# Output transposes moved from the matrix engine to 32 by 32 squares on VectorE, and half of the squarings moved to ScalarE

## What is computed

```python
out = np.einsum('hk,bskhg->bshg', softmax(weight), x_unf)      # 7 taps, causal
x1  = (sigmoid(x @ w_gate) * (x @ w_val)) @ w_out              # d_ff 1536
h   = x1 @ w_in2;  r = np.maximum(h, 0);  y = (r * r) @ w_out2 # d_ff 2048
```

## Time and profile before

| | |
|---|---|
| median of 3 executions | 2421.84 us |
| profiled execution, whole | 2421.73 us |
| profiled execution, span of the trace | 2419.5 us |
| TensorE busy | 2387.3 us, 99% |
| VectorE busy | 1824.4 us, 75% |
| ScalarE busy | 1162.6 us, 48% |
| GpSimd busy | 174.6 us, 7% |
| TensorE's granted clock, mean | 0.998 |

### The profile page before, as it was taken

How to read it: one execution, slowest core, us unless ns; L and a number is a source line. 1 busy time by engine, 2 the same in 40 slices (tenths; PEclk the granted TensorE clock), 3 DMA queues, 4 the chain that set the end, 5 groups by cost and what they waited for, 6 DMA issues and landing times.

```text
span 2419.5 us, 54234 instructions
## 1 busy us (share of the span) xinstructions
PE 2387.3 (99%) x20880; PEld 1942.8 (80%) x20880; DVE 1824.4 (75%) x3468; ACT 1162.6 (48%) x2208; POOL 174.6 (7%) x164
## 2 busy tenths in 40 slices
PE   6999999999999999999999999999999999999998
PEld 5788888888888888888888888888888888888886
DVE  6777777777777777877777777778777777777755
ACT  3544544454544444544545444445445444454544
POOL 3300000000000000000000000000000000000010
PEclk9999999999999999999999999999999999999999
DMA  5211111111111101111111111111111111111110
GB/s 131 60 47 28 39 48 30 46 28 41 46 42 36 45 22 46 48 30 46 28 41 46 31 45 36 33 46 48 30 46 28 39 48 30 46 28 41 40 38 19
DMA packets 99902, 99.41 MB, mean 41 GB/s; under 512 B 8736, under 2 KB 86048, under 8 KB 99872
## 3 DMA queue, kind: packets, MB, share of 16 engines
q1 hardware_dynamic: 99856, 98.99, 16.7%
q10 hardware_dynamic: 16, 0.00, 0.0%
HBM read 19.27 MB, written 12.58 MB: 13 GB/s over the span
## 4 chain that ended last, share of the span: by engine, by line
PE 98%; DVE 1%; ACT 0%; issue 0%; DMA 0%; POOL 0%; SPq 0%; ACTq 0%; DVEq 0%
PE hp L400 53%; PE acc L466 25%; PE acc L471 17%; PE hp L401 1%; DVE y L815 1%; PE acc L467 0%; PE hp L506 0%; PE acc L472 0%; DMA stage<-in_moe_w_val_dram 0%; PE hp L515 0%; POOL wo L358 0%; DVE hid_t L767 0%; DMA moved<-z_parts 0%; SPq L263 0%; ACT xT L637 0%
## 5 line engine op out<-in xcount | busy, mean ns | idle before, releaser
L400 PE MATMUL hp<-xs,w 64*128 64x512 f32 x5760 | 1413.2, 389 | 13.6 <-DVE hid_t L767 5.3
L401 PE MATMUL hp<-xs,w 64*128 64x512 f32 x5760 | 1413.2, 389 | 0.0
L400 PEld LDWEIGHTS hp<-xs,w 64*128 64x128 f32 x5760 | 1061.7, 185 | 256.1 <-DVE hid_t L767 7.3
L401 PEld LDWEIGHTS hp<-xs,w 64*128 64x128 f32 x5760 | 1061.7, 185 | 0.0
L781 DVE TENSOR_TENSOR lo<-hid_t,hi 128x512 fp32r<-128x512 f32 x896 | 615.4, 687 | 7.9
L771 DVE TENSOR_TENSOR hid_t<-act_t 128x512 f32<-128x512 f32 x512 | 384.7, 752 | 246.1 <-ACT act_t L628 246.1
L625 ACT ACTIVATE act_t<-hp 128x512 f32<-128x512 f32 x384 | 229.9, 599 | 689.4 <-PE hp L400 689.3
L467 PE MATMUL acc<-hi,wo 64*128 64x512 f32 x1792 | 560.7, 393 | 0.0
L466 PE MATMUL acc<-hi,wo 64*128 64x512 f32 x1792 | 560.7, 393 | 0.0
L767 DVE TENSOR_TENSOR hid_t<-hp,act_t 128x512 f32<-128x512 f32 x384 | 265.0, 690 | 261.7 <-ACT act_t L625 253.3
L628 ACT ACTIVATE act_t<-hp 128x512 f32<-128x512 f32 x512 | 302.8, 598 | 310.6 <-PE hp L401 310.6
(11 more groups left out here) (69 smaller groups left out, 1890.3 us busy)
## 6 DMA issues: line engine op xcount, KB each, us to landing
xs<-xs SPq DMA_DIRECT2D x160, 256.0 KB, 3.8
xs<-y_rest SPq DMA_DIRECT2D x128, 128.0 KB, 3.1
out_dram<-stage SPq DMA_DIRECT2D x32, 384.0 KB, 2.6
xin<-in_x_dram SPq DMA_DIRECT2D x30, 384.0 KB, 4.3
moved<-y_parts SPq DMA_DIRECT2D x32, 128.0 KB, 2.2
moved<-z_parts SPq DMA_DIRECT2D x64, 64.0 KB, 2.0
stage<-in_moe_w_out_dram SPq DMA_DIRECT2D x7, 384.0 KB, 4.2
stage<-in_moe_w_in_dram SPq DMA_DIRECT2D x12, 128.0 KB, 2.9
```

The costliest lines, as they stand in the source:

```text
L400: low = pe.matmul(hp[:, 2 * pair, :], w[lower, wk, c], xs[lower, xk, :], start=s, stop=e)
L401: up = pe.matmul(hp[:, 2 * pair + 1, :], w[upper, wk, c], xs[upper, xk, :], start=s, stop=e)
```

## The change

**VectorE turns the output.** For every block but the last, 24 VectorE transposes of 32 partitions by 4 squares of 32 (`o_squares`, `turn_z`) write `o_sb` directly. In `gated` they stand three to a tile in t = 4 to 11, in the one `squared` that follows another `squared` two to a tile in t = 4 to 15. TensorE's transposes, ScalarE's copies and the shifted PSUM pairs go; the last block is turned as before (`turn_last`). The store of a block waits for all its 24 squares (`o_turned`).

**ScalarE squares the odd tiles** of the second MLP (`square_odd`), VectorE the even ones.

**Smaller edits.** EARLY goes from 4 to 3: a convolution tap moves from `gated` to `squared`, and the 32 input squares are spread over 9 tiles in place of 8. `cross_z` is one transfer of 64 by 512 in place of two of 64 by 256, and GpSimd's addition (`add_z_rest`) one instruction in place of two. `in2` of pair 0 behind a gated stage waits for product 10 only, of pair 1 for product 11.

```diff
-    EARLY = 4
+    EARLY = 3
+        o_squares = []
+        for c in range(D // Q):
+            of, ch = (z, slice(c * Q, (c + 1) * Q)) if c < P // Q else (z_parts, slice(c * Q - P, (c + 1) * Q - P))
+            for m in range(P // Q):
+                tok = slice(m * Q, (m + 1) * Q)
+                o_squares.append((of[ch, :].rearrange("c (b s) -> c b s", b=B)[:, :, tok],
+                                  o_sb[tok, :, c * Q:(c + 1) * Q]))
...
             def store(j):
-                sp.wait_ge(turn_copied, 4 * j + 4)
+                if isinstance(j, int) and j == NB - 1:
+                    sp.wait_ge(turn_copied, 4)
+                else:
+                    sp.wait_ge(o_turned, O_SQUARES * (j + 1))
                 sp.dma_start(out_v[bass.ds(j * P, P), :, :], o_sb).then_inc(o_room, 16)
...
             def gated(j, prev):
...
-                    if prev and prev[0] == 2 and t == TR1:
-                        turn(prev[1], (prod_done, T1 * j + t))
...
+            def square_odd(j, t, prev):
...
+                act.wait_ge(relu_done, T2 * j + t + 1)
+                act.activation(hid_t[:, t % 4, :], act_t[:, t % 2, :], ACT.Square).then_inc(odd_sq_done, 1)
...
-                    if t == TR1 + 1 and prev and prev[0] == 2:
-                        turn_copy(prev[1])
...
+            def turn_z(j, part, parts):
+                if part == 0:
+                    dve.wait_ge(o_room, 16 * (j + 1))
+                    dve.wait_ge(z_added, 2 * j + 1)
+                for n in range(part * O_SQUARES // parts, (part + 1) * O_SQUARES // parts):
+                    if n == REST_SQUARES:
+                        dve.wait_ge(z_rest_done, j + 1)
+                    src, dst = o_squares[n]
+                    dve.transpose(dst, src).then_inc(o_turned, 1)
...
+                    if t >= 4 and prev and prev[0] == 2:
+                        turn_z(prev[1], t - 4, T1 - 4)
...
-                    hidden(2, j, t, prev)
+                    if t >= 4 and prev[0] == 2:
+                        turn_z(prev[1], t - 4, T2 - 4)
+                    if t % 2 == 0:
+                        hidden(2, j, t, prev)
```

More of the change, by code:

```diff
@@ L165, in conv_gated_squared_mlp @@
         z_added = sem("z_added")
+        o_turned = sem("o_turned")
         def inward1(k, c0, n):
@@ L219, in column_of @@
             return q // 2 + T2P * (q % 2)
[L221 to L226, removed]
         def x0_home(j):
@@ L288, in cross_z @@
             def cross_z(j):
-                sp.wait_ge(z_added, 2 * j + (1 if isinstance(j, int) and j == NB - 1 else 2))
-                sp.dma_start(z_moved[lower, :, :], z_blocks[upper, :, 0, :]).then_inc(z_crossed, 16)
-                sp.dma_start(z_moved[upper, :, :], z_blocks[lower, :, 1, :]).then_inc(z_crossed, 16)
+                if isinstance(j, int) and j == NB - 1:
+                    sp.wait_ge(z_added, 2 * j + 1)
+                    sp.dma_start(z_moved[lower, :, :], z_blocks[upper, :, 0, :]).then_inc(z_crossed, 16)
+                    sp.dma_start(z_moved[upper, :, :], z_blocks[lower, :, 1, :]).then_inc(z_crossed, 16)
+                else:
+                    sp.wait_ge(z_added, 2 * j + 2)
+                    sp.dma_start(moved[lower, :], z_parts[upper, :]).then_inc(z_crossed, 16)
             def store(j):
-                sp.wait_ge(turn_copied, 4 * j + 4)
+                if isinstance(j, int) and j == NB - 1:
+                    sp.wait_ge(turn_copied, 4)
+                else:
+                    sp.wait_ge(o_turned, O_SQUARES * (j + 1))
                 sp.dma_start(out_v[bass.ds(j * P, P), :, :], o_sb).then_inc(o_room, 16)
@@ L371, in add_z_rest @@
             def add_z_rest(j):
[L372 to L376, removed]
+                pool.wait_ge(z_crossed, 16 * (j + 1))
+                nc.gpsimd.tensor_tensor(z_parts[lower, :], z_parts[lower, :], moved[lower, :], ALU.add) \
+                    .then_inc(z_rest_done, 1)
             for n in range(len(pieces)):
@@ L423, in in1 @@
             def in1(j, t, prev):
-                turns = prev and prev[0] == 2
                 if t == 0:
@@ L427, in in1 @@
                     pe.wait_ge(x0_spread, 64 * j + 64)
-                if t < 2 and turns:
+                if t < 2 and prev and prev[0] == 2:
                     pe.wait_ge(relu_done, T2 * prev[1] + T2 - 2 + 2 * t)
[L430 to L433, removed]
                 else:
@@ L437, in in1 @@
                     pe.wait_ge(w_lo, split_upto[SECOND_HALF])
-                low, up = into(pair1(t, prev), w1, x0_home(j), columns(t))
+                low, up = into((t % 2), w1, x0_home(j), columns(t))
                 low.then_inc(gate_ready, 1)
@@ L444, in in2 @@
                     pe.wait_ge(x1_spread, 48 * j + 48)
[L445 to L452, removed]
+                if p < 2 and prev[0] == 1:
+                    pe.wait_ge(prod_done, T1 * prev[1] + T1 - 1 + p)
                 else:
                     pe.wait_ge(relu_done, T2 * j + 2 * p - 2)
-                low, up = into(pair2(p, prev), w2, x1_home(j), columns(p))
+                low, up = into(p % 2, w2, x1_home(j), columns(p))
                 low.then_inc(hid_ready, 1)
@@ L491, in out2, with turn_last @@
                 outward(wo2, column_of(t), t % RING, t == 0, t == T2 - 1, *room(prev)).then_inc(out2_done, 1)
-            def turn(j, free):
-                last = isinstance(j, int) and j == NB - 1
+            def turn_last(j):
                 a, b = hp[:, 0, :], hp[:, 1, :]
[L498 to L502, removed]
+                pe.wait_ge(relu_done, T2 * NB)
+                pe.wait_ge(z_added, 2 * j + 2)
                 pe.sem_inc(turn_begun, 1)
@@ L507, in turn @@
                     mm = pe.transpose(b[:, to], z[upper, columns(n)], ident[upper, upper])
[L508 to L512, removed]
+                mm.then_inc(turned, 1)
+                a, b = hp[:, 2, :], hp[:, 3, :]
+                pe.wait_ge(z_rest_done, j + 2)
+                pe.sem_inc(turn_begun, 1)
                 for g in range(B // 2):
@@ L516, in turn @@
                     mm = pe.transpose(b[:, to], z_blocks[upper, g, 1, :], ident[upper, upper])
-                mm.then_inc(turned, 1 if last else 2)
+                mm.then_inc(turned, 1)
             def turn_x(j):
@@ L588, in _ @@
             some_of(rest_)
-            turn(NB - 1, (relu_done, T2 * NB))
+            turn_last(NB - 1)
         @block.scalar
@@ L612, in round_hi, with squared_upto @@
                 else:
[L613 removed]
+                    squared_upto(j, t)
                     act.copy(hi[:, t % RING, :], hid_t[:, t % 4, :]).then_inc(hi2_done, 1)
+            def squared_upto(j, t):
+                act.wait_ge(odd_sq_done if t % 2 else even_sq_done, T2P * j + t // 2 + 1)
+            def square_odd(j, t, prev):
+                if t >= 4:
+                    act.wait_ge(lo2_done, T2 * j + t - 3)
+                elif prev[0] == 1:
+                    act.wait_ge(lo1_done, T1 * prev[1] + T1 - 3 + t)
+                else:
+                    act.wait_ge(lo2_done, T2 * prev[1] + T2 - 3 + t)
+                act.wait_ge(relu_done, T2 * j + t + 1)
+                act.activation(hid_t[:, t % 4, :], act_t[:, t % 2, :], ACT.Square).then_inc(odd_sq_done, 1)
             def activate(kind, j, t, prev):
                 if t >= 2 or (prev and prev[0] == kind):
[L618 to L619 removed]
+                    if kind == 1:
+                        act.wait_ge(prod_done, T1 * j + t - 1)
+                    elif t >= 2:
+                        squared_upto(j, t - 2)
+                    else:
+                        squared_upto(prev[1], T2 - 2 + t)
+                elif prev and prev[0] == 1:
+                    act.wait_ge(prod_done, T1 * prev[1] + T1 - 1 + t)
                 elif prev:
[L621 to L622 removed]
+                    squared_upto(prev[1], T2 - 2 + t)
                 if kind == 1:
                     act.wait_ge(gate_ready, T1 * j + t + 1)
[L625 removed]
+                    act.activation(act_t[:, t % 2, :], hp[:, 2 * (t % 2), :], ACT.Sigmoid).then_inc(sig_done, 1)
                 else:
                     act.wait_ge(hid_ready, T2 * j + t + 1)
[L628 removed]
+                    act.activation(act_t[:, t % 2, :], hp[:, 2 * (t // 2 % 2) + t % 2, :], ACT.Relu) \
                        .then_inc(relu_done, 1)
@@ L673, in turn_copy @@
             def turn_copy(j):
-                last = isinstance(j, int) and j == NB - 1
                 act.wait_ge(o_room, 16 * (j + 1))
-                act.wait_ge(turned, 2 * j + (1 if last else 2))
+                act.wait_ge(turned, 1)
                 for half in range(2):
@@ L679, in turn_copy @@
                              hp[:, half, 0:B * R].rearrange("p (b d) -> p b d", b=B)).then_inc(turn_copied, 1)
-                if last:
-                    act.wait_ge(turned, 2 * j + 2)
+                act.wait_ge(turned, 2)
                 for half in range(2):
```

(10 more changed lines are left out.)

20 lines of the change are left out of this document (9 added, 11 removed).

## The result

The changed kernel takes 2717.28 us (median of 4 executions, 2715.34 to 2718.76) against 2421.53 us before (median of 4, one execution more than above), a ratio of 1.122 (95% interval 1.120 to 1.124): 12% slower, 296 us. The forecast was 2687, in a range of 2600 to 2750.

A forecast was written before the change was run, and what follows sets the result against it. TensorE, 99% busy, was taken as the bound. 29 rounds x (7.5 late start + 1.5 clock) = 261, plus 4.5 for the last gated stage, minus 0.5, made +265 on 2421.7: 2687 us, range 2600 to 2750.

The forecast's parts named there:

- The queue: SyncE's queue: x1's spreads stand behind a store awaiting all 24 squares, so the squared stage begins 7.5 us later each round.
- E: End of the last output square in the gated stage; bounds 627.1 and 630.5, taken as 630.0.
- the store's bytes: The store's 384 KB run just ahead of the spreads and could delay them 0 to 2.7 us; 0.45 taken.
- the walk: VectorE's gated-stage work from 598.29 summed without idle time: 32.3 us, giving 630.5 for the last square's end.
- VectorE's pace: In the gated stage VectorE, with output squares at 0.333 us each, is slower than TensorE and sets the last square's end.
- rival 1: Squares are cheap and TensorE keeps the pace in the gated stage: +4.6 + 1.5 us a round, 2603 us; chance 0.08.
- The stall beside GpSimd: VectorE stalls when GpSimd works beside it; in the gated stage it falls on a remainder instead, already counted.
- The clock: TensorE's idle gap before each squared stage makes its clock fall: 1.5 us a round, with 0 and 3.0 as ends.
- Rival 4: The clock stays up behind TensorE's gaps: 29 x 7.5 + 3.5 - 0.5 = 220, 2642 us; chance 0.12.
- TensorE's saving: Removing the output turn between two pairs of matmuls saves TensorE 0.52 us each, 31 times: 16.1 us.
- Rival 3: Only VectorE's lateness counts, not the queue: TensorE waits at `out1(9)`, net 0.6 us a round, 2438 us; chance 0.03.
- Rivals 2 and 5: First: spread lands in time, 2405.6 us, chance 0.03. Second: store and spreads share engines fully, clock low longer, 2813 us, 0.08.

The follow-up runs named there:

- run 1: Changed kernel with SyncE issuing the three spreads of x1 ahead of the store that waits for the squares: 2431.15 us, ratio 1.004.
- run 2: Kernel before, with only the store of blocks 0 to 29 waiting for the gated stage's last product instead of ScalarE's copies: 2651.58 us, ratio 1.096.
- run 14: Not a follow-up run: "run" is a verb here, and 14 of TensorE's pairs run from 779.47 to 785.45 in the changed kernel.
- run 3: Changed kernel with 26 pairs of idle matmuls on TensorE during the wait for x1: 2659.68 us, ratio 1.099.
- run 5: Changed kernel with output squares spread, one per tile in gated t = 4 to 11, 16 in squared t = 9 to 15, store a round later: 2405.48 us.
- runs 6 and 7: All squarings of the squared stage back on VectorE: in the kernel of run 5 2404.46 us, in the kernel of run 1 2431.29 us.
- run 8: Kernel with all 24 output squares in the squared stage from t = 4, with all squarings back on VectorE: 2473.02 us, ratio 1.021.
- runs 4 and 8: First: changed kernel, 24 output squares moved to the squared stage, store a round later, behind the spreads: 2420.73 us. Second: that kernel, all squarings on VectorE: 2473.02 us.
- run 9: Kernel of run 5 with the convolution tap back in the gated stage (EARLY = 4): 2405.07 us, ratio 0.993.

## Why the prediction was right, step by step

A loop round grew from 74.2 to 84.3 us in the mean, by 10.1 us; the forecast had 9.0.

**The queue** (added: 7.5 us a round; measured 7.8). The mechanism is shown from both sides: run 1 takes the wait off the spreads and 286 us go, run 2 adds only a late store to the kernel before and 231 us come. Both of its parts came out near their terms. E was taken as 630.0 and was 629.8. From E to the stage's start I took 6.4 us, it was 6.9: the store went out 0.29 us behind the last square, not at once, and the third spread landed 4.8 and not 4.3 us behind its issue. The term for the store's bytes (0.45) was thus about right, that for the queue's own step was missing. That E came out within 0.2 us is in part luck: the walk added up 32.3 us and the trace has 31.5 (656.78 to 688.29), in part because product and remainder take 1.2 and not 1.33 us where a tap follows. The step from the walk's 630.5 down to 630.0 had no term of its own.

**VectorE's pace.** Squares at 0.333 us were right, which leaves rival 1 out. The stall beside GpSimd fell where it was expected, on a remainder: 1.46 us at 674.40, beside this row of GpSimd.

```profile
674.03 1.28 POOL L379 TENSOR_TENSOR xs<-y_parts,xs 64x512 fp32r<-64x512 f32 x1 [13.71 <-ACT xs L669]
```

**The clock** (1.5 us a round; measured 2.3 in the mean). This is the one term that was clearly too small. I read it from the row of a gap of 2.6 us, where the clock fell after TensorE had started again, and took one value for all rounds. Behind the gaps of the changed kernel it was low from the first pair on, and the number of slow pairs was not the same: counted over the timeline, they cost 1.4 to 1.5 us in 8 of the 29 rounds, 2.2 to 2.4 in 9 and 2.7 to 2.9 in 12. The round shown above is one of the 9. The start of the stage and the first pair at full pace, in one of the 8 and in one of the 12:

```profile
611.66 0.79 PE L409 MATMUL hp<-xs,w 64*128 64x512 f32 x1 [7.42 <-DMA xs<-xs]
...
614.72 0.39 PE L409 MATMUL hp<-xs,w 64*128 64x512 f32 x1
```

```profile
779.47 0.79 PE L409 MATMUL hp<-xs,w 64*128 64x512 f32 x1 [7.40 <-DMA xs<-xs]
...
785.45 0.39 PE L464 MATMUL acc<-hi,wo 64*128 64x512 f32 x1
```

From 611.66 to 614.72 run 7 pairs, 1.45 us more than 0.23 each; from 779.47 to 785.45 run 14, 2.8 us more, behind the same gap. My 1.5 was the least of these values and not their mean. What decides between them was not tried. 29 x 0.8 = 23 us of the 30 us between 2687 and 2717 are this; the longer way from E to the stage's start is 29 x 0.3 = 9 more. Rival 4 is out: no round is without slow pairs, and run 3 shows that they come from the idle time. The Trainium skill (TensorE: Matmul & The Clock Gate, HAM oscillation) says that such a cost is paid in each round; this trace agrees, with 1.4 us or more in each of the 29.

**TensorE's saving** (0.52 us x 31 = 16.1) was real, and invisible in the changed kernel, where TensorE only waited longer. Run 5 shows it: 2421.4 - 2405.5 = 15.9 us.

**Rival 3** (VectorE's lateness alone, 2438 us) was no rival but the second layer: run 1 lays it bare at 2431 us. The lateness a round is (2431.2 - 2421.0 + 16.1) / 29 = 0.9 us, against 1.1 in the forecast, which put all of it at `out1(9)`, where run 1 has 0.5. **Rivals 2 and 5** did not come.

**The squarings** were priced at nothing; runs 6 and 7 show that for two arrangements, and run 8 that the cover has an end: 52 us / 29 = 1.8 us a round (51 us if runs 4 and 8 are each taken against the kernel before on their own chip). The moved tap costs nothing either in run 9's arrangement; in the changed kernel itself it wasn't tried. Nor were the single transfer of `cross_z` and the earlier start of `in2`; they stay unpriced.

## What to carry to other kernels

When a transfer's wait is tied to a later event, look at what is issued behind it in the same queue: what moves is not one transfer but all that follow. Before moving work to an engine with idle time, find the place in the stage where it will stand and who waits for what comes behind; kernels with the same 24 transposes came out 296 us slower, 10 us slower, the same, or 16 us faster, by the transposes' place and the queue's order. And price a wait on TensorE with the clock's fall added, as a range: here it was 1.4 to 2.9 us behind gaps of one length, and a single gap told only the least of it.

## What the runs showed of the hardware

The length of the gap alone does not set what a fallen clock costs. Behind 1.4 us (run 3) the clock stayed up; behind 2.6 and 2.8 us it fell once, at a cost of 1.5 us, and once not the earlier trace rows; behind 5.9 us (run 2) it cost 1.5 us a round; behind 7.3 to 7.7 us it cost 1.4 to 2.9 us, with a mean of 2.3. I had not expected that issuing the third spread would take 1.08 us in place of 0.61 when the store ran just ahead. Run 2 has the same (1.06), and run 1, where no store runs ahead, has 0.61; what sets it was not tried.
